# Window attention and two fused FFNs: work of the first chunks moved between VectorE and GpSimd

## The reference

```
w = softmax(weight_gen, over the 7 taps)
x = for each token and head: sum over 7 taps of w * x_pad   # 2 x 4096 x 192
h = x @ w_in1;  g = h * cos(h);            x = g @ w_out1   # 192 -> 2048 -> 192
h = x @ w_in2;  g = max(0.01 * h, h);      out = g @ w_out2
```

## Time and profile before

| | us |
|---|---|
| median of 3 runs | 1144.72 (1144.63 to 1144.95) |
| the profiled execution's own time | 1145.67 |
| its span in the profile | 1143.9 |
| PE busy (share of the span) | 1129.4 (99%) |
| DVE busy | 932.0 (81%) |
| ACT busy | 723.1 (63%) |
| POOL busy | 88.8 (8%) |

### The profile page before, as it was taken

One profiled execution on the slowest core, in us unless ns is written; L12 is line 12 of the kernel. 1 busy time (PEld: TensorE's weight loads), 2 busy tenths in 40 slices (PEclk: granted clock), 3 DMA queues, 4 the chain that ended last, 5 costly groups with the idle time before them and its releaser, 6 DMA issues.

```text
span 1143.9 us, 22933 instructions
## 1 busy us (share of the span) xinstructions
PE 1129.4 (99%) x9766; PEld 996.5 (87%) x9766; DVE 932.0 (81%) x911; ACT 723.1 (63%) x775; POOL 88.8 (8%) x82
## 2 busy tenths in 40 slices
PE   7999999999999999999999999999999999999998
PEld 5778888888988888898888988889899998988986
DVE  7999897988979899697896969879797896978443
ACT  6766775757657576574755757566575655757544
POOL 6860000000000000000000000000000000000000
PEclk9999999999999999999999999999999999999999
DMA  9760201102011110301103011020201102010001
GB/s 256 209 127 1 63 1 40 38 14 64 1 42 36 31 48 1 77 1 36 43 1 77 1 39 40 15 63 1 59 20 32 46 1 77 1 38 6 1 15 29
DMA packets 85262, 48.41 MB, mean 42 GB/s; under 512 B 58156, under 2 KB 78762, under 8 KB 84776
## 3 DMA queue, kind: packets, MB, share of 16 engines
q1 hardware_dynamic: 80712, 41.70, 14.3%
q0 software_dynamic: 4448, 5.24, 2.4%
HBM read 35.12 MB, written 11.80 MB: 41 GB/s over the span
## 4 chain that ended last, share of the span: by engine, by line
PE 91%; DVE 3%; ACT 1%; issue 1%; ACTq 0%
PE slot L1213 42%; PE acc_a L1213 29%; PE acc_b L1213 18%; DVE g_lo L913 1%; DVE gate L1027 1%; ACT gate L793 0%; PE acc_b L1186 0%; PE acc_a L1179 0%; PE acc_b L1187 0%; PE acc_a L1178 0%; PE acc_a L1177 0%; DVE x_a_lo L941 0%; ACT g_hi L730 0%; ACT taps_w L856 0%; DVE gate L908 0%
## 5 line engine op out<-in xcount | busy, mean ns | idle before, releaser
L1213 PE MATMUL acc_a<-g_hi,out_hi_lo 64*128 64x512 f32 x2000 | 696.3, 388 | 0.0
L913 DVE TENSOR_TENSOR g_lo<-gate,g_hi 128x1024 fp32r<-128x1024 f32 x251 | 307.9, 1227 | 121.5 <-ACT g_hi L730 121.4
L1213 PEld LDWEIGHTS acc_a<-g_hi,out_hi_lo 64*128 64x128 f32 x2000 | 367.8, 184 | 26.1
L1213 PE MATMUL acc_b<-g_hi,out_hi_lo 64*128 64x512 f32 x1000 | 388.4, 388 | 1.3 <-DVE g_lo L913 1.2
L1213 PE MATMUL acc_a<-g_lo,out_hi_lo 64*128 64x512 f32 x1000 | 386.5, 386 | 0.0
L1213 PE MATMUL acc_b<-g_lo,out_hi_lo 64*128 64x512 f32 x1000 | 386.4, 386 | 0.0
L730 ACT ACTIVATE g_hi<-gate 128x1024 fp32r<-128x1024 f32 x251 | 266.2, 1061 | 107.7 <-PE acc_b L1213 86.0
L1213 PE MATMUL slot<-x_a_hi,in_a_lo 64*128 64x512 f32 x1024 | 301.0, 388 | 1.6 <-DVE g_lo L927 1.2
L1213 PE MATMUL slot<-x_b,in_b_hi 64*128 64x512 f32 x1024 | 300.6, 387 | 0.5 <-DVE x_b L951 0.2
L1213 PE MATMUL slot<-x_a_lo,in_a_hi 64*128 64x512 f32 x1024 | 300.3, 387 | 0.0
L1213 PE MATMUL slot<-x_a_hi,in_a_hi 64*128 64x512 f32 x1024 | 300.1, 386 | 0.0
(11 more groups left out here) (110 smaller groups left out, 1023.8 us busy)
## 6 DMA issues: line engine op xcount, KB each, us to landing
x_win<-in_x SPq DMA_DIRECT2D x14, 960.0 KB, 4.8
x_columns<-prods SPq DMA_DIRECT2D x56, 96.0 KB, 2.0
out<-turned_a SPq DMA_DIRECT2D x240, 16.0 KB, 1.5
x_raw_a<-x_columns SPq DMA_DIRECT2D x14, 256.0 KB, 2.9
out<-turned_b SPq DMA_DIRECT2D x120, 16.0 KB, 1.5
result<-x_columns SPq DMA_DIRECT2D x14, 128.0 KB, 3.0
out_raw<-in_moe_w_out SPq DMA_DIRECT2D x3, 512.0 KB, 9.7
out_hi_lo<-in_moe_w_out POOLq DMA_DIRECT2D x2, 768.0 KB, 10.2
```

The source lines that it names most:

```text
L913: nc.vector.tensor_tensor(g_lo[:, q % 2, :], result_of(i, q), g_hi[:, q % 2, :].bitcast(FP32), ALU.subtract)\
L1213: return nc.tensor.matmul(to, w[rows, :], x[rows, :], start=start, stop=stop)
```

## The change

Three things are moved, and nothing is added or left out of the arithmetic.

- Number 9 of chunk 1's attention, `add(0, 0, 1)`, goes from DVE to POOL, right behind number 7. Number 8, the product apart, is issued by DVE after step 4 instead of step 5 (`APART_STEP`), and now waits for its window itself. `add_apart` stays on DVE in step 6.
- The softmax parts of chunk 2 go from step (1, 0) to the ends of steps (0, 2), (0, 3) and (0, 4).
- POOL issues three of the second weights' DMAs ahead of its wait for `att` 22, subtracts `in_a` right behind the low part of unit (0, 7), `in_b` behind that of unit (1, 0), and each of the four pairs behind the low part of one of the units (1, 1) to (1, 4).

```diff
-        ATT_POOL, ATT_END = 8, 5
+        ATT_POOL, APART_STEP, ATT_END = (0, 1, 2, 3, 4, 5, 6, 7, 9), 4, 6
...
             if c == 1:
-                yield lambda: product(0, APART, 0, J).then_inc(apart, 1)
+                def product_apart():
+                    engine.wait_ge(own_loaded[1], 16)
+                    wait_for_halo()
+                    product(0, APART, 0, J).then_inc(apart, 1)
+
+                yield product_apart
...
-        SOFT_AT = {}
+        SOFT_AT = {(0, 2): [(2, "sum")], (0, 3): [(2, "guard"), (2, "invert")], (0, 4): [(2, "multiply")]}
...
-            of_pool = list(attention(1, pool))[:ATT_POOL]
+            of_chunk_1 = list(attention(1, pool))
+            of_pool = [of_chunk_1[n] for n in ATT_POOL]
...
-            pool.wait_ge(att, 2 * ATT_STEPS)
-            out_lows(3)
             pool.dma_start(W2.in_a_hi[:, :], w_in2[0:DA, :]).then_inc(w2_hi_loaded[0], 16)
             pool.dma_start(W2.in_b_hi[0:DB, P:], w_in2[DA:dim, :]).then_inc(w2_hi_loaded[1], 16)
             pool.dma_start(W2.in_b_hi[DB:P, 0:hidden], w_in2[DA:dim, :]).then_inc(w2_hi_loaded[1], 16)
+
+            pool.wait_ge(att, 2 * ATT_STEPS)
+            out_lows(3)
...
-            pool.wait_ge(lo_ready, unit(1, 0) + 1)
+            pool.wait_ge(lo_ready, unit(0, 7) + 1)
...
             every = slice(0, hidden)
+            pool.wait_ge(lo_ready, unit(1, 0) + 1)
...
-            for f in OUT_PIECES:
+            for n, f in enumerate(OUT_PIECES):
+                pool.wait_ge(lo_ready, unit(1, n + 1) + 1)
...
-                if (i, step) == (0, ATT_END + 1):
-                    for instruction in of_chunk_1[ATT_POOL + 1:]:
-                        instruction()
+                if (i, step) == (0, ATT_END):
+                    of_chunk_1[10]()
...
-                    for part in TAIL_PARTS:
-                        softmax(2, part)
                     product(1, 0)
...
-                if step == ATT_END:
-                    of_chunk_1[ATT_POOL]()
+                if step == APART_STEP:
+                    of_chunk_1[8]()
```

## The result

| | before | after |
|---|---|---|
| median, us | 1144.88 (6 runs, 1144.63 to 1145.09) | 1148.75 (6 runs, 1147.39 to 1149.61) |
| profiled execution, us | 1145.67 | 1148.88 |
| its span, us | 1143.9 | 1147.1 |
| PE busy | 1129.4 (99%) | 1130.2 (99%) |
| DVE busy | 932.0 (81%) | 934.6 (81%) |

The ratio is 1.0032, 95% interval 1.0022 to 1.0042: the change makes the kernel 3.9 us slower. On the 1144.72 from which the prediction started that is 1148.4, just inside the upper end of its range (the median itself lies 0.15 above it).

The account below looks back on a forecast made before the run. PE was taken as the bound, with standstills in the first 90 us that wait for DVE. Terms of +2.5 - 0.1 - 0.1 - 0.65, say +1.7, and about +0.5 for the clock took 1144.72 to 1146.9 us; range 1143.4 to 1148.6.

Parts of the forecast that it names:

- The guard is held up: On DVE beside POOL's first `add_pairs`: asked at about 38.7, the guard ends only at 40.12, costing up to 1.3 us.
- The multiply: On DVE, softmax of chunk 2: asked at 44.0, held by POOL's product to 44.9, ended at 45.3.
- the product apart: On DVE, asked at 45.22: waits for POOL's second `add_pairs` to 48.54 and ends at 49.50.
- PE's block: The block that fills unit 7 starts at 51.95 instead of 47.61, 4.34 us later.
- Without the clock: The sum of the terms before the clock's price: +2.5 - 0.1 - 0.1 - 0.65 = +1.65 us, say +1.7.
- The pieces: POOL's second weights, 64 to 90 us: PE gets back 0.65 us at 88.07 and 0.1 at 74.47.
- not slower: Rival: guard not held up, or product apart in ahead of the second `add_pairs`; about -0.9 us, 1143.8, chance 0.34.
- the term for TensorE's clock: PE, idle from 47.9 to 51.95, may lose its full clock: 1.0 - 0.6, about +0.5 us.
- the clock stays down longer: Rival: as forecast, with the clock's whole price of 3.7 us, up to 1150.1; chance within the forecast's 0.58.
- then DVE's own chain takes over: From `add_apart` at 54.06 to the sums, DVE's 6.98 us decide: sums at 61.04, +2.5 us.
- slower: Whole kernel's time above 1147.0 us: chance 0.34, half of the forecast's cases and the unseen.
- costs nothing here: POOL's addition ends at about 51.2, and DVE comes to `add_apart` only at 54.06: no cost.

Follow-up runs that it names:

- no_guard: The changed kernel without the guard of chunk 2 (the addition of 1e-9): 1143.93 us, 0.9995 of the kernel before.
- multiply_later: The changed kernel with chunk 2's softmax multiply one step later, at the end of step (0, 5): 1144.05 us, 0.9995 of the kernel before.
- apart_step5: The changed kernel with the product apart back at step 5: 1143.88 us, 0.9990 of the kernel before.
- busy_pe: The changed kernel with 18 pairs of zero-weight matmuls in PE's wait ahead of the block filling unit 7: 1146.65 us, 1.0015 of the kernel before.
- pieces_alone: The kernel before with only POOL's second weights in pieces and their DMAs issued earlier: 1146.98 us, 1.0015 of the kernel before.
- softmax_back: The changed kernel with chunk 2's four softmax parts put back into step (1, 0): 1146.32 us, 1.0009 of the kernel before.
- add_back: The changed kernel with the addition back on DVE, ahead of `add_apart` in step 6: 1147.96 us, 1.0026 of the kernel before.
- softmax_in_gap: The changed kernel with chunk 2's sum at (0, 3) and its guard, invert and multiply in (0, 7): 1144.97 us, 0.9997 of the kernel before.
- softmax_alone: The kernel before with only chunk 2's four softmax parts moved up: 1145.51 us, 1.0004 of the kernel before.

## Why the prediction was right, and where it was off

**Right, step by step.**
- *The guard is held up*: asked at 38.7, free at 40.12 was the reckoning, 38.61 to 40.28 the row. Its fraction at 40.58 (40.5), the product of unit 4 at 42.87 (42.87).
- *The multiply* ended at 45.44 (45.3); *the product apart* at 49.58 (49.50), behind a second `add_pairs` that had asked 0.09 us sooner. no_guard, multiply_later and apart_step5 each break one link, and the wait of 4 us goes or shrinks to under 0.9.
- *PE's block* at 51.91 (51.95), `add_apart` at 54.12 (54.06), no late start ahead of the transposes.
- *Without the clock*: the sum said +1.65 us; busy_pe measures 1146.65 - 1144.99 = 1.66, its sums at 61.20 (61.04). The +1.7 of the working stands. That the two agree to 0.01 us is chance: the interval of that ratio, 1.0006 to 1.0024, spans 0.7 to 2.7 us.
- *The pieces*: the 0.65 us at 88 came back, and the 0.1 at 74.47 was 0.17.
- *The rival "not slower"* (1143.8, chance 0.34) is what the kernels without the meeting give: 0.9995 twice, about 1144.1, within an interval of some 1 us to either side. It was a fair price for the other side of that point.

**Off: the term for TensorE's clock.** The prediction put it at "1.0 - 0.6, about +0.5"; it measures 2.1 us by the medians and 2.47 in the traces. Both halves were wrong.
- The 1.0 came from "a low stretch of 2 us, a guess nearer to 0 since work resumes at once". The granted clock is 0.50 for all of 51 to 57, and the pairs run at the low rate from 51.91 to 57.20, 5.3 us. 12 of the 19 starts of the block come 0.42 us or more after the one before instead of 0.23, some 2.5 us. The beginning of the fall was forecast from the earlier trace rows; the end of it had no row. The rival "the clock stays down longer", bound 3.7 us, is what came, at over half of its bound.
- The 0.6 was credit for DVE being the later one at the sums. It weighed PE, which does stand idle 0.34 us ahead of the sums in busy_pe, against DVE, and left out ACT: the low part of unit 6 also waits for ACT's `g_hi`, and in ACT's program that stands behind the three copies of what PE's transposes deliver. In the kernel before this path had 1.0 us to spare: `g_hi` ended at 56.20, DVE's `x_b` at 57.22. Without the fall of the clock PE's transposes come 3.73 us later than there and `add_apart` 2.61, so nothing is left of it. First the row of the kernel before, then those of busy_pe:

```profile
55.14 1.06 ACT L730 ACTIVATE g_hi<-gate 128x1024 fp32r<-128x1024 f32 x1
```

```profile
58.83 1.06 ACT L738 ACTIVATE g_hi<-gate 128x1024 fp32r<-128x1024 f32 x1
...
59.14 0.69 DVE L959 TENSOR_TENSOR x_b<-slot,x_b 64x512 fp32r<-64x512 f32 x1
59.92 1.23 DVE L921 TENSOR_TENSOR g_lo<-gate,g_hi 128x1024 fp32r<-128x1024 f32 x1
```

  `g_hi` ends at 59.89, `x_b` at 59.83: the two paths are level, and the step "then DVE's own chain takes over" was no cover. What PE's transposes lose, the sums lose in full: from the transposes to the sums are 4.81 us in both kernels (58.86 to 63.67, 56.39 to 61.20).

With the measured 2.1 in place of 0.5 the sum is 1144.7 + 1.7 + 2.1 = 1148.5. The time fell on the side "slower", for which the text had 0.34, by the size of this one term. That it still lies within the range is partly luck: the range was said to leave out the long stay at the low clock, the stay came, and what is left to the upper end is 0.2 us, less than the runs of the changed kernel differ among themselves (1147.39 to 1149.61).

**Not seen: one part that needs another.** The prediction priced the pieces by the low parts that they spare and asked what the softmax gives at (1, 0): "ACT's sine is what the product there waits for". It didn't ask what the pieces would do to the softmax had it stayed: pieces_alone and softmax_back cost about 1.7 and 1 us over the kernel before. The total was not touched, since the change moves both, but the forecast of softmax_back failed on it.

**The addition "costs nothing here".** True, and shown by add_back. The text's other sentence, "if DVE were early, it would be what `add_apart` waits for", is softmax_in_gap: 2.74 us of waiting.

## What to carry to other kernels

Before a small instruction is put into a gap of VectorE, ask what GpSimd does in that very stretch, and which instructions stand behind it: 0.18 us of work in the wrong place pushed two others to a later turn and made 3.7‰ of difference (1.0032 against 0.9995 without it), and with the last of the three one step later (apart_step5) it cost nothing. A wait of TensorE like the one here, 4 us, must be priced at more than itself: here the work behind it ran at half the clock for 5.3 us and lost 2.5, and that is only covered if the other engines' chain has slack at the next meeting point: look for it row by row. And when parts of a change are tested singly, a part that loses alone may be one that only needs its partner.

## What the runs showed of the hardware

- **Three instructions of one SBUF operand, same place, same neighbour.** At 38.6 us, while POOL's `add_pairs` (36.7, 3.52 us) is in: the sum, a reduction, takes 0.38 us (softmax_in_gap), the reciprocal 0.34 (no_guard), and the guard, an addition of a constant, 1.65 to 1.72 in all kernels that have it there (0.18 when alone). All three are small and read one operand; only the last is held up. The Trainium skill, page "SBUF — State Buffer", section "Who interferes with whom", says this: `tensor_scalar` can take the port pair that VectorE shares with GpSimd, `tensor_reduce` on trn2 never does. The trace agrees with both. On the reciprocal that section says nothing; no_guard shows it free.
- **The low clock outlasts the wait.** PE's last pair before it starts at 47.45, the granted clock is 0.74 from 50 to 51 and 0.50 from 51 to 57, though PE is at work again from 51.91. Late starts of up to 0.85 us at the same place (no_guard), and of 1.15 elsewhere (softmax_back), left the stretches at 1.00.
- **A standstill can be slack.** The product apart stood 1.3 us too long in the kernel before, and a delay of 1.7 us ahead of it (softmax_alone) moved its end by 0.3.
- **The hold goes both ways.** GpSimd's two products of 768 elements take 3.06 us together in the changed kernel and 3.78 in softmax_in_gap, where DVE's product apart (42.89 to 44.52) asks while the first of them is in and gets its turn between the two. In no_guard it gets in behind the second of them and ahead of `add_pairs`. In each case the one that had waited went next, also against an engine that issued without a break.
